# Token rows kept in token order and gathered once per expert tile, instead of scattered by expert during attention

## What is computed

```python
# attention: q, k, v are (8, 8, 576, 64); no softmax
kv = np.einsum('bhsd,bhse->bhde', k, v)
out = np.einsum('bhsd,bhde->bhse', q, kv)
rms = np.sqrt(np.mean(out * out, axis=-1, keepdims=True) + 1e-06)
x = (out / rms * g_norm)            # turned into 4608 token rows of 512
# top-1 experts: 8 experts, F = 1024
logits = x @ w_gate + modality_bias[modality_id]
e_idx = np.argmax(logits, axis=1)   # gate_w: softmax value of the chosen expert
h = np.maximum(x[mask] @ w1[e], 0.0)
out[mask] = gate_w[mask, None] * (h @ w2[e])
# GLU: d_ff = 1536
gate = 1.0 / (1.0 + np.exp(-(x @ w_gate)))
return (gate * (x @ w_val)) @ w_out
```

## Time and profile before

| | us |
|---|---|
| median of 3 runs | 1572.0 |
| the profiled execution, its own time | 1571.37 |
| its span in the trace | 1569.7 |
| PE busy (matmuls) | 1445.6 (92%) |
| DVE busy | 861.7 (55%) |
| ACT busy | 437.3 (28%) |
| POOL busy | 333.5 (21%) |

### The profile page before, as it was taken

One profiled execution on the slowest core, in us unless ns is written; L12 is line 12 of the kernel. 1 busy time (PEld: TensorE's weight loads), 2 busy tenths in 40 slices (PEclk: granted clock), 3 DMA queues, 4 the chain that ended last, 5 costly groups with the idle time before them and its releaser, 6 DMA issues.

```text
span 1569.7 us, 25868 instructions
## 1 busy us (share of the span) xinstructions
PE 1445.6 (92%) x8548; PEld 1187.0 (76%) x8549; DVE 861.7 (55%) x1463; ACT 437.3 (28%) x766; POOL 333.5 (21%) x414
## 2 busy tenths in 40 slices
PE   5666649999999999997989999999999999999997
PEld 4554437888888888886777888888888888888886
DVE  3445366546653666434677555655565555755551
ACT  4444312222222222223443112422233222422222
POOL 0222454444443444421210000100010000100001
PEclk8766559999999999998999999999999999999999
DMA  9565134325342444215995733273441744234411
GB/s 334 191 237 192 72 135 123 101 86 159 123 128 59 125 133 146 76 46 148 349 339 218 197 141 141 74 218 145 146 163 53 215 150 165 86 121 159 167 62 42
DMA packets 95311, 234.03 MB, mean 149 GB/s; under 512 B 18686, under 2 KB 43262, under 8 KB 89088
## 3 DMA queue, kind: packets, MB, share of 16 engines
q1 hardware_dynamic: 73280, 190.96, 36.7%
q0 software_dynamic: 17216, 39.75, 7.7%
q10 hardware_dynamic: 4736, 2.26, 0.7%
HBM read 179.47 MB, written 54.54 MB: 149 GB/s over the span
## 4 chain that ended last, share of the span: by engine, by line
PE 82%; DVE 5%; issue 4%; DMA 4%; ACT 2%; another core or an unknown queue 1%; SPq 1%; POOL 0%; POOLq 0%; DVEq 0%; ACTq 0%
PE ps L1415 29%; PE ps L1395 17%; PE ps L1361 14%; PE ps L1339 14%; PE ps L1291 2%; PE ps L1348 2%; DMA mixes<-mix 2%; PE ps L1278 1%; PE ps L1385 1%; PE ps L1255 1%; DMA graw<-in_moe_w_val 1%; DMA vt<-in_v 1%; ACT qp L669 0%; DVE a_lo L1161 0%
## 5 line engine op out<-in xcount | busy, mean ns | idle before, releaser
L1415 PE MATMUL ps<-a_hi,st 128*128 128x512 f32 x1344 | 421.4, 389 | 0.9 <-DVE u L1200 0.9
L1415 PEld LDWEIGHTS ps<-a_hi,st 128*128 128x128 f32 x1344 | 252.3, 188 | 54.0 <-DVE a_lo L1161 1.5
L1395 PE MATMUL ps<-wo,shi 128*128 128x512 f32 x864 | 268.6, 392 | 7.1 <-DVE slo L1170 6.3
L1415 PE MATMUL ps<-a_lo,st 128*128 128x512 f32 x672 | 261.4, 389 | 0.0
L1339 PE MATMUL ps<-ew,xhi 128*128 x640 | 202.5, 398 | 3.1 <-DVE xlo L1029 1.8
L1361 PE MATMUL ps<-ew,hhi 128*128 x640 | 197.1, 389 | 1.3 <-DVE hlo L1046 1.3
L1395 PEld LDWEIGHTS ps<-wo,shi 128*128 128x128 f32 x864 | 162.4, 189 | 45.3 <-issue 5.1
L614 POOL DMA_INDIRECT out<-ot,out_tok x36 | 35.9, 998 | 717.7 <-ACT ot L765 711.9
L1395 PE MATMUL ps<-wo,slo 128*128 128x512 f32 x432 | 170.0, 393 | 0.0
L1415 PEld LDWEIGHTS ps<-a_lo,st 128*128 128x128 f32 x672 | 126.1, 188 | 26.2
L1361 PEld LDWEIGHTS ps<-ew,hhi 128*128 128x128 f32 x640 | 120.1, 188 | 26.4 <-issue 1.5
(11 more groups left out here) (194 smaller groups left out, 1907.4 us busy)
## 6 DMA issues: line engine op xcount, KB each, us to landing
st<-mixes SPq DMA_DIRECT2D x48, 1792.0 KB
raw<-in_moe_w SPq DMA_DIRECT2D x64, 512.0 KB
mixes<-mix SPq DMA_DIRECT2D x24, 512.0 KB, 8.5
xg<-x_rows POOLq DMA_DIRECT2D x160, 64.0 KB
kt<-in_k SPq DMA_DIRECT2D x8, 1152.0 KB, 5.9
vt<-in_v SPq DMA_DIRECT2D x8, 1152.0 KB, 9.4
qt<-in_q SPq DMA_DIRECT2D x8, 1152.0 KB, 5.9
mixes<-gv SPq DMA_DIRECT2D x12, 768.0 KB, 6.5
```

Source lines behind the costliest of these rows:

```text
L1395: last = mm(ps[:, 4 + m, :], s[:, rows], wo[f // 2][:, w, f % 2], start=(f == 0 and w == 0 and s is shi[slot]), stop=(f == GC - 1 and s is ...
L1415: last = mm(bank_of(f, idx), st[f % 2][:, at:at + 128], x[:, idx, k, :], start=(k == 0 and w == 0 and x is a_hi), stop=(k == 1 and w == 1))
```

## The change

- **xb and x_rows.** DVE writes a slot's normed rows to a ring of 8 columns (4 slots), after the logits now. SP stores them in token order, with two plain DMAs to a slot (four where the slot spans two batches: 80 in all) of 128 pieces of 1 KB each. The store of slot o stands in SP's order one slot behind the norm, between the loads of the batches. DVE waits for the store of slot o-4 before it writes slot o. The 72 indirect DMAs and the zero rows are gone.
- **Groups.** Four groups (24, 24, 16, 8 columns) instead of nine.
- **The list.** DVE turns each place into a row within a tile (spot_r) and a number of a tile (spot_q). For every pair of columns, hot_row makes a one-hot matrix of 128 x 128 that holds the token number at the row (bf16, in two parts); POOL makes 64 of these during attention and DVE the last 8. After the totals, DVE makes the one-hot matrices of the tile numbers (hot_q), and PE multiplies them: 72 products of 128 x 43 give the list of token numbers, one column for each tile (L1410 of the changed kernel). One more product gives the same list in the order in which a tile's rows come out (turn_f).
- **Tiles.** POOL copies a column of the list, gathers the tile's 128 rows of 2 KB by one indirect DMA into a single buffer xs (gather_x), and ACT moves xs to xg by four DMAs from SBUF to SBUF (load_x). POOL's gather waits until the tile before has left xs. ACT's load_x of tile t+2 stands behind h_of of tile t. The loads of token numbers are gone.
- compact_rows stands behind the second tile's turn, gate_values behind the first's, and four products keep PE going instead of three.

```diff
 
     LAG_T, LAG_OUT, LAG_NORM, LAG_LG = 1, 3, 4, 5
...
     ENDS = [(c + m) // 2 - 1 for c, m in GROUPS]
     assert sum(m for _, m in GROUPS) == T and T == 2 * S
...
-    x_rows = nc.dram_tensor("x_rows", [2 * E * CAP, XW], F32, kind="Internal").ap()
+    x_rows = nc.dram_tensor("x_rows", [N, D], F32, kind="Internal").ap()
...
+        def hot_row(engine, k, part):
+
+            return engine.tensor_scalar(hot[:, k, part], across[:], spot_r[:, k:k + 1], tok_part[:, part, k:k + 1], ALU.is_equal, ALU.mult)
...
-            for b in range(BATCH):
+            def load_kv(b):
                 wait(sp, pe_kv, b - 1)
                 load(kt, k_v, b, k_in)
                 load(vt, v_v, b, v_in)
-                if b >= 2:
-                    sp.wait_ge(qp_made, (J * (b - 1) + 1) // 2)
-                load(qt, q_v, b, q_in)
-                if 1 <= b <= EARLY:
-                    load_raw(sp, 0, b - 1)
+
+            def store(o):
+                sp.wait_ge(x_normed, 2 * o + 2)
+                at, b, j = 2 * o % RING, 2 * o // J, 2 * o % J
+                for n in range(2):
+                    part = slice(R * n, R * n + R)
+                    if spans_two(o):
+                        sp.dma_start(x_v[b, n, :, j], xb[part, at]).then_inc(x_out[o % (RING // 2)], 16)
+                        sp.dma_start(x_v[b + 1, n, :, 0], xb[part, at + 1]).then_inc(x_out[o % (RING // 2)], 16)
+                    else:
+                        sp.dma_start(x_v[b, n, :, j:j + 2], xb[part, at:at + 2]).then_inc(x_out[o % (RING // 2)], 16)
+
+            load_kv(0)
+            load(qt, q_v, 0, q_in)
+            load_kv(1)
+            load(qt, q_v, 1, q_in)
+            load_raw(sp, 0, 0)
+            load_kv(2)
+            for s in range(S + LAG_NORM + 1):
+                for b in range(2, BATCH):
+                    if s == (J * (b - 1) + 1) // 2:
+                        sp.wait_ge(qp_made, s)
+                        load(qt, q_v, b, q_in)
+                        if b <= EARLY:
+                            load_raw(sp, 0, b - 1)
+                        if b + 1 < BATCH:
+                            load_kv(b + 1)
+                o = s - LAG_NORM - 1
+                if o >= 0:
+                    store(o)
             for unit in range(EARLY, UNITS):
                 load_raw(sp, 0, unit)
...
-            for g, (c0, m) in enumerate(GROUPS):
-                pool.wait_ge(idx_made, g + 1)
-                for c in range(c0, c0 + m):
-                    nc.gpsimd.indirect_dma_start(
-                        out=x_rows, out_offset=bass.IndirectOffsetOnAxis(ap=r_idx[:, c:c + 1], axis=0),
-                        in_=xb[:, c % RING, :], in_offset=None).then_inc(x_out[g], 16)
-
-            for g, (c0, m) in enumerate(GROUPS):
-                pool.wait_ge(x_out[g], 16 * m)
+            pool.wait_ge(iota_made, 12)
+
+            pool.wait_ge(pair_made, 1)
+            for g, (c0, m) in enumerate(GROUPS[:LAST]):
+                pool.wait_ge(spot_made, g + 1)
+                for k in range(c0 // 2, (c0 + m) // 2):
+                    for part in range(2):
+                        last = hot_row(nc.gpsimd, k, part)
+                last.then_inc(hot_made, 1)
+
+            for n in range(RING // 2):
+                pool.wait_ge(x_out[n], stored(S - RING // 2 + n))
...
-            def row_of(t):
-                return pool.value_load(x_row[0:1, bass.ds(t.n, 1)], min_val=0, max_val=E * CAP - 128)
-
-            def load_x(t, row=None):
-                when(xt_made, t.n - 1)
-                row = row_of(t) if row is None else row
-                for g in range(4):
-                    src = x_v[bass.ds(row, 128), g // 2, 128 * (g % 2):128 * (g % 2) + 128]
-                    nc.gpsimd.dma_start(xg[32 * g:32 * g + 32, t.p], src.rearrange("(t j) x -> j t x", j=32)).then_inc(x_in[t.p], 16)
-
-            def load_tok(t):
-                row = row_of(t)
-                nc.gpsimd.dma_start(tok_now[:, t.p:t.p + 1], tok_v[bass.ds(row, 128)], allow_slow_non_contiguous=True).then_inc(t_in[t.p], 16)
+            def gather_x(t):
+                if not isinstance(t.n, int) or t.n > 0:
+                    when(x_in[1 - t.p], 64 * (t.half + t.p))
+                nc.gpsimd.tensor_copy(tok_x[:], tok_of[:, bass.ds(t.n, 1)]).then_inc(aimed, 1)
+                when(aimed, t.n + 1)
+                nc.gpsimd.indirect_dma_start(
+                    out=xs[:], out_offset=None, in_=x_rows,
+                    in_offset=bass.IndirectOffsetOnAxis(ap=tok_x[:], axis=0)).then_inc(sorted_in, 16)
 
...
+            pool.wait_ge(list_made, 1)
+            for n in range(2):
+                gather_x(Tile(0, n))
             pool.wait_ge(tables_made, 1)
-            pool.wait_ge(pads_out[1], 16 * (E - 1))
             use = Use(pool)
-            load_x(Tile(0, 1))
             pool.wait_ge(gates_out, 16)
+            pool.wait_ge(list_made, 4)
...
-                use(Tile(i, c + 2), load_x)
+                use(Tile(i, c + 2), gather_x)
                 if c > 1:
                     use(Tile(i, c - 2), scatter)
-                use(Tile(i, c), load_tok)
-                if c > 0:
-                    use(Tile(i, c - 1), gather_gate)
+                use(Tile(i, c), gather_gate)
...
+            def load_x(t):
+                wait(act, xt_made, t.n - 1)
+                act.wait_ge(sorted_in, 16 * t.n + 16)
+                for g in range(4):
+                    act.dma_start(xg[32 * g:32 * g + 32, t.p],
+                                  xs[:, 128 * g:128 * g + 128]).then_inc(x_in[t.p], 16)
...
+                use(Tile(i, c + 2), load_x)
+
+            load_x(Tile(0, 0))
+            load_x(Tile(0, 1))
...
-                nc.vector.tensor_scalar(r_idx[:, c0:c0 + m], r_p[:, 0:m], 2.0, half[:], ALU.mult, ALU.add).then_inc(idx_made, 1)
+                pairs = slice(c0 // 2, (c0 + m) // 2)
+                for n in range(2):
+                    part = slice(R * n, R * n + R)
+                    then(nc.vector.tensor_copy(spot_i[part, pairs], r_p[part, 0:m].rearrange("p (k two) -> p k two", two=2)[:, :, n]))
+                then(nc.vector.tensor_scalar(spot_qi[:, pairs], spot_i[:, pairs], 7, None, ALU.logical_shift_right))
+                nc.vector.scalar_tensor_tensor(out=spot_r[:, pairs], in0=spot_qi[:, pairs], scalar=-128.0, in1=spot_i[:, pairs],
+                                               op0=ALU.mult, op1=ALU.add).then_inc(spot_made, 1)
+                then(nc.vector.tensor_copy(spot_q[:, pairs], spot_qi[:, pairs]))
+                then(nc.vector.tensor_tensor(past[:, pairs], spot_q[:, pairs].unsqueeze(2).to_broadcast([128, m // 2, E - 1]),
+                                             edge_i[:, 1:E].unsqueeze(1).to_broadcast([128, m // 2, E - 1]), ALU.is_ge))
...
-                    if 2 * o >= RING:
-                        old = group_of(2 * o - RING)
-                        dve.wait_ge(x_out[old], 16 * GROUPS[old][1])
...
-                    for jj in range(2):
-                        nc.vector.tensor_tensor(
-                            xb[:, 2 * o % RING + jj, 0:D // 2].rearrange("p (g h i) -> p h g i", g=2, h=PAIRS),
-                            outs(o)[:, :, jj, 0:DH].rearrange("p h (g i) -> p h g i", g=2),
-                            scale[:, :, jj].unsqueeze(2).unsqueeze(3).to_broadcast([128, PAIRS, 2, 32]), ALU.mult).then_inc(x_normed, 1)
                     g = group_of(2 * o)
                     wait(dve, pe_lg, g - 1)
                     at = 2 * o - GROUPS[g][0]
                     nc.vector.tensor_tensor(lgh[:, g % 2, :, at:at + 2, :], outs(o)[:, :, :, DH:KX],
                                             scale.unsqueeze(3).to_broadcast([128, PAIRS, 2, E]), ALU.mult).then_inc(lgh_made, 1)
+                    if o >= RING // 2:
+                        dve.wait_ge(x_out[o % (RING // 2)], stored(o - RING // 2))
+                    for jj in range(2):
+                        nc.vector.tensor_tensor(
+                            xb[:, 2 * o % RING + jj].rearrange("p (g h i) -> p h g i", g=2, h=PAIRS),
+                            outs(o)[:, :, jj, 0:DH].rearrange("p h (g i) -> p h g i", g=2),
+                            scale[:, :, jj].unsqueeze(2).unsqueeze(3).to_broadcast([128, PAIRS, 2, 32]), ALU.mult).then_inc(x_normed, 1)
...
-            dve.wait_ge(idx_made, len(GROUPS))
-            nc.vector.memset(r_unit[:], 1.0)
-            nc.vector.memset(split_to[:], UNITS // 2).then_inc(exp_asked, 1)
-            dve.wait_ge(pe_counts, 1)
-            nc.vector.tensor_scalar(pad_row[:], ps[0:1, 3, TOTAL], 1.0, None, ALU.add).then_inc(pads_made, 1)
...
-            then(nc.vector.tensor_tensor_scan(r_end[:], r_unit[:], r_nt[:], 0.0, ALU.mult, ALU.add))
-
+            then(nc.vector.tensor_scalar(step[:], r_nt[:, 0:E - 1], float(-QE), None, ALU.add))
+            then(nc.vector.tensor_tensor(moved[:], past[:], step[:].unsqueeze(1).to_broadcast([128, KP, E - 1]), ALU.mult))
```

(44 more changed lines are left out.)

126 lines of the change are left out of this document (72 added, 54 removed).

## The result

The changed kernel takes 1548.0 us (median of 4, 1545.9 to 1554.1); the kernel before, run beside it, takes 1571.5 (4 runs, 1569.7 to 1574.7). The ratio is 0.9855 [0.9822, 0.9887], so 23 us are gained where 47 were forecast. The profiled execution took 1545.9, span 1544.1, which is 25.6 us under the span of before.

A forecast was written before the change was run, and what follows sets the result against it. PE bounds the expert and GLU stages; in the first 249 us scatters starve it. 61.2 - 8 + 5 - 4 - 7.1 = 47.1 us off 1571.4 gives 1524.3, stated as 1525; range 1503 to 1547, to 1556 with most rivals.

The forecast's parts named there:

- Term 1: Attention slots: without POOL's scatters PE gets its instructions, and eight slots take 33.7 us instead of 94.87, gain 61.2 us.
- Term 2: Attention slots: DVE waits for stores queued behind loads on SP before reusing the ring, 8 us lost, between 0 and 24.
- the ring binds: Rival: each store waits for the whole group of loads, 36 us lost instead of 8, 1553 us; chance 0.17.
- Term 3: DVE and POOL during attention: fewer groups gain 5 us, POOL's 64 one-hot products lose 4 us.
- Term 4: First expert tiles: list products, gathers and moves put the second tile 43.5 instead of 36.4 us after last logits, 7.1 lost.
- The expert stage: Steady expert tiles: nothing changes; the later load of tile t+2 still leaves 2.2 us to spare.
- The other side: Rival: 9216 small row writes, not POOL's issue, starve PE, so the 61 us come back, 1578 to 1586 us; chance 0.08.

The follow-up runs named there:

- e1: Kernel before, its 72 scatters replaced by plain stores in token order on SP's queue, old ring and groups kept: 1519.8 us, against 1574.6 for the kernel before.
- e14: e9 with one change, the nine groups of before instead of four: 1537.0 us, against 1521.3 for the kernel before beside it.
- e9: Changed kernel with a ring of 12 columns instead of 8: 1528.5 us, against 1573.3 for the kernel before beside it.
- e15: Kernel before, unaltered, run as a kernel of its own on a fifth chip: 1521.5 us, against 1521.9 for the same kernel beside it.
- e3: Changed kernel whose stores take their bytes from a constant tile, so DVE never waits for a store: 1532.3 us, against 1574.6 for the kernel before.
- e13: Changed kernel with a ring of 12 columns, its four groups and e11's transition: 1524.0 us, against 1521.3 for the kernel before beside it.
- e8: Changed kernel with the nine groups of before instead of four: 1547.0 us, against 1575.4 for the kernel before beside it.
- e10: Changed kernel without the 64 one-hots on POOL, one memset by DVE instead: 1545.4 us, against 1573.3 for the kernel before beside it.
- e4: Changed kernel with ACT making tile 0's high part before loading tile 1's rows: 1543.7 us, against 1574.6 for the kernel before beside it.
- e11: Changed kernel with second gather buffer free of warm-up, tile 0's high part before tile 1's moves, compact_rows before tile 0's turn, low part before gate values: 1541.9 us.
- e17: e13's kernel again, on a sixth chip: 1521.7 us, against 1575.0 for the kernel before beside it.
- e2: e1 with the 72 scatters issued again on POOL, indices out of bounds so they move no row: 1581.9 us, against 1574.6 for the kernel before.
- e16: Changed kernel, unaltered, on the same chip as e15: 1549.1 us, against 1521.9 for the kernel before beside it.

## Why the prediction was wrong

The sign was right, but the gain was forecast at twice its size, 47.1 us for 23.5. The forecast's own range, 1503 to 1547, missed the 1548.0; only the wider one with the rivals, to 1556, held it. Two terms of the sum were too good, and a third had a part that was priced too low: the scatters (9.4 us), the ring (6.4), and one-hots, places and list (3.9). The last root was to come 54.2 us earlier (61.2 - 8 + 5 - 4) and came 36.3 earlier. A row of kernels between the two splits this: 209.9 before, 158.1 with plain stores and the old ring (e1), 166.0 with the change's list, places and one-hots, still nine groups, and a ring of 12 (e14), 159.2 with four groups (e9), 173.6 with a ring of 8 (the changed kernel). From e14 on each step is one edit. The profiles are of several chips, so each step is good to some 3 us.

| step | forecast | measured on the last root |
|---|---|---|
| scatters go | +61.2 | +51.8 |
| one-hots, places, list | -4 (POOL) | -7.9 |
| four groups for nine | +5 | +6.8 |
| ring of 8 | -8 | -14.4 |
| sum | +54.2 | +36.3 |
| transition to the last down | -7.1 | -7.9 |

To the last down 28.4 us were gained. The last part, as said, took 2.8 back, and the profiled execution lies 2.1 below the median of its runs: 23.5.

**Term 1, the mechanism right, the size 9 us off.** "Four of them hold a batch's k'v products. Undisturbed, such a slot takes 5.12": in e1 these four take 7.8, 6.1, 9.2 and 7.9 us, 31.0 instead of 20.5 (8.7, 7.0, 8.6 and 7.1 in e15, scatters and all). The row it was taken from, 145.51 to 150.63, was the shortest of its kind. The batch's k and v had been issued at 121.1 and 121.6 us, ahead of a burst, and the k'v products start at 145.78, only 0.27 us behind the root, with the slot's other products all but done; in e1's slots at 57.98 and 127.88 us they start 1.6 us behind it. In e1 only the hole of 3.18 us is seen for itself; the DMA engines are full in two of the four slots (1.03 and 1.04) and not in the others (0.43 and 0.33), so the loads alone don't explain the rest. The other four came out as forecast (12.2 us for 13.2).

**Term 2, the step whose reasoning failed.** The store's landing (12.4 us at most) was about right. "DVE needs it three slots on, which is 3 x 3.31 to 3.31 x 2 + 5.12, 10 to 12 us" was not: I let DVE run at a mean pitch. Ahead of the three longest waits the three slots take 7.6, 7.4 and 6.6 us, and one of these stretches had 7.4 us in the trace of before too (roots at 75.12, 77.30, 79.56 and 82.51). The rival "the ring binds" had 36 us; 14.4 were lost, since some 10 of the 26.6 us of waiting cost nothing (e3).

**Term 3.** The groups were right within 2 us, but only with a ring that doesn't bind (e14 against e9 and e13). In the changed kernel itself they are worth 1.6 at most, within the noise (e8). POOL's operations took 0.79 us, above my upper end of 0.60, and cost nothing that e10 could show; so the 7.9 us between e1 and e14 are rather DVE's six added operations per group, which I had counted inside the groups' gain, and the order of its writes, which I had not counted. That last point is argued, not shown: no run takes these parts singly, and e14's ring is also shorter than e1's. The Trainium skill's rule on the shared port pair (SBUF — State Buffer, "Who interferes with whom") cost no measurable time here.

**Term 4, right in size, by other parts.** The 72 list products took not 8 us but 3, as the line's view shows them within 3.5 us (64 in 2.50 us in one piece, 39 ns each):

```profile
L1410 PE MATMUL ps<-hot_q,hot x72: 194/208/218, 186.6 to 190.0; 128*128 128x43 bf16 x72
```

Those 5 us, and 1.7 more, were lost again, most of it in ACT's order (4.3 us for the second up by e4), which I had not read. Timeline of ACT in the changed kernel:

```profile
195.49 11.39 ACTq L755 DMA_DIRECT2D xg<-xs  x8
208.08 0.62 ACT L761 CAST xhi<-xt 128x512 fp32r<-128x512 f32 x1 [17.64 <-issue]
```

and of DVE there:

```profile
199.69 0.71 DVE L1107 STREAM_TRANSPOSE xt<-xg 128x512 f32<-128x512 f32 x1 [3.72 <-DMA xg<-xs]
...
208.73 0.69 DVE L1112 TENSOR_TENSOR xlo<-xt,xhi 128x512 fp32r<-128x512 f32 x1 [6.83 <-ACT xhi L761]
209.34 0.70 DVE L1107 STREAM_TRANSPOSE xt<-xg 128x512 f32<-128x512 f32 x1
209.97 0.13 DVE L1091 SCALAR_TENSOR_TENSOR r_spare<-r_nt,r_all 128x8 f32<-128x8 f32 x1
```

Tile 0 is turned at 200.4, but its high part stands in ACT's queue behind the moves of tile 1, and these wait for the second gather. Second up at last logits + 45.2 instead of 43.5, before 36.4. e11 wins back 6.3 of the 7.9 us (508.8 to the last down), e17 all of it (507.3).

**The expert stage** kept its 11.8 us per tile (third and fourth up at + 57.6 and + 69.4 from the last root); no tile waits for its rows, and one tile is 2.2 us late (1.0 before) at a place where DVE waited 0.7 us for a weight piece. **The other side** ("the waits stay") had a slower kernel, for the wrong reason: row writes were cleared by e2, but on the chip of e15 and e16 there were no such waits to remove, and the change is 27 us slower. On the chip of e13 and e14 before takes 1521 us too; no profile of it was taken there. The profile of one chip could not tell this; it is the gravest thing the forecast left out.

## What to carry to other kernels

Size a ring by the shortest run of slots in which its stores fall due, not by the mean pitch; here four columns more, of 1 KB per partition each, brought the last root forward by 14 us, and another queue for the same stores by 3. When a batch of work is moved, walk every in-order engine across the seam: both losses at the first tile were an instruction that was ready and stood behind one that was not. And where the gain rests on "the engine waits for nothing that the trace shows", take the kernel before on more than one chip: a ring of 12 with e11's transition runs in 1522 to 1524 us on either kind, 3.4% under the kernel before on one and 0.2% above it on the other.

## What the runs showed of the hardware

- Indirect DMAs issued by POOL starve PE on some chips, or in some sessions. With the DMA engines at 0.06, PE got 45 products in 11 us while POOL issued six empty scatters; on four of the six chips of the table, and in the first comparison, the kernel before takes 1570 to 1579 us, on the other two 1516 to 1526, with the same scatter of 0.96 us every 1.27. The Trainium skill (Runtime: NRT & Kernel Launch, "Instruction fetch mechanics") says that fetching is hidden by the rate of issue; if fetching is what stalls here, which no row names, the trace speaks against it; the fetching packets themselves take about 1 us on either kind.
- Even without starving, the 144 k'v products of batch 4 have one hole of 3.2 to 3.3 us of idle "issue" behind the first 84 (e1, e15).
- A bfloat16 product of 128 rows by 43 columns costs 39 ns in a row of 64, each with its own weight load beside it.
- A one-hot tensor_scalar of 128 x 128 (float32 in, bfloat16 out, two scalars from SBUF) takes 0.79 us on POOL and 0.34 on DVE. Between POOL's copy of an index and the gather that uses it lie 0.8 to 0.9 us.
